# Expert and feed-forward layers of a fused attention and mixture-of-experts kernel: transposes by DMA and VectorE in place of the matmul engine, and the experts' second layer two blocks behind the first

## The reference

```
x = attention(q, k, v, a_re, a_im)              # decayed linear attention, 4 x 768 tokens, 8 heads of 48: x is 3072 x 384
e = argmax(x @ w_gate); gate = softmax(x @ w_gate)[e] * sigmoid(x @ w_output_gate)[e]     # 8 experts
y = gate * (relu(x @ w1[e]) @ w2[e])            # 384 -> 1024 -> 384, each token through one expert
h = y @ w_in;  out = max(0.01 * h, h) @ w_out   # 384 -> 2048 -> 384, all tokens
```

## Time and profile before

| | us |
|---|---|
| median of 3 runs (lowest, highest) | 1001.77 (1001.34, 1003.72) |
| the profiled execution's own time | 1002.58 |
| its span, first to last instruction | 1000.6 |
| PE busy | 949.9 (95%) |
| DVE, ACT, POOL busy | 412.9, 454.2, 509.5 |

### The profile page before, as it was taken

How to read it: one execution, slowest core, us unless ns; L and a number is a source line. 1 busy time by engine, 2 the same in 40 slices (tenths; PEclk the granted TensorE clock), 3 DMA queues, 4 the chain that set the end, 5 groups by cost and what they waited for, 6 DMA issues and landing times.

```text
span 1000.6 us, 17624 instructions
## 1 busy us (share of the span) xinstructions
PE 949.9 (95%) x5980; PEld 846.0 (85%) x5981; DVE 412.9 (41%) x742; ACT 454.2 (45%) x772; POOL 509.5 (51%) x429
## 2 busy tenths in 40 slices
PE   6999999999839999999999999999999999999997
PEld 5778788888727999998998989999999999999996
DVE  6889988988824323333232322212112122112111
ACT  7999889996612222222222333333333333333322
POOL 4235665665547558568839943243343332433433
PEclk9999999999968999999999999999999999999999
DMA  4643454320342343253535520010010010000000
GB/s 145 174 136 104 148 171 130 118 81 28 100 169 95 109 166 120 85 167 115 154 106 165 189 57 17 16 40 16 9 40 17 24 32 17 32 1 1 32 1 32
DMA packets 47192, 84.06 MB, mean 84 GB/s; under 512 B 23813, under 2 KB 36377, under 8 KB 44569
## 3 DMA queue, kind: packets, MB, share of 16 engines
q1 hardware_dynamic: 40984, 48.59, 16.3%
q0 software_dynamic: 6144, 34.65, 9.9%
HBM read 65.80 MB, written 17.38 MB: 83 GB/s over the span
## 4 chain that ended last, share of the span: by engine, by line
PE 74%; ACT 10%; DVE 5%; issue 5%; POOL 5%; SPq 1%; DMA 1%; POOLq 0%; DVEq 0%; ACTq 0%
PE bank L2127 20%; PE bank L2140 20%; PE bank L2085 11%; PE bank L2107 10%; POOL wm L1866 3%; PE bank L2095 2%; PE bank L1096 2%; DVE neglog L848 1%; PE bank L1178 1%; PE bank L1136 1%; POOL wm L1864 1%; PE bank L1164 1%; PE bank L1138 1%; PE bank L1106 1%; PE bank L1119 1%
## 5 line engine op out<-in xcount | busy, mean ns | idle before, releaser
L1894 POOL TENSOR_TENSOR act_r<-act_f,act_r 128x512 fp32r<-128x512 f32 x96 | 124.6, 1298 | 260.3 <-ACT act_r L1955 257.6
L2140 PE MATMUL bank<-w_out_r,act_r 128*128 128x384 f32 x1152 | 217.7, 337 | 0.3 <-POOL act_r L1894 0.3
L2127 PE MATMUL bank<-x,w_in_r 128*128 128x512 f32 x864 | 216.7, 395 | 0.0
L2140 PEld LDWEIGHTS bank<-w_out_r,act_r 128*128 128x128 f32 x1152 | 204.8, 188 | 8.8 <-POOL act_r L1894 0.6
L2016 DVE TENSOR_TENSOR act_f<-bank,small 128x512 f32<-128x512 f32 x96 | 66.5, 693 | 292.7 <-ACT small L1952 275.2
L2127 PEld LDWEIGHTS bank<-x,w_in_r 128*128 128x128 f32 x864 | 159.6, 188 | 29.5
L1952 ACT ACTIVATE small<-bank 128x512 f32<-128x512 f32 x96 | 57.5, 599 | 191.2 <-PE bank L2127 191.1
L2085 PE MATMUL bank<-wm,x_tr 128*128 (+1 forms) x522 | 129.5, 402 | 4.0 <-POOL wm L1866 1.7
L2107 PE MATMUL bank<-wm,h_tr 128*128 (+1 forms) x696 | 128.6, 339 | 0.7 <-DVE h_tr L2000 0.7
L2107 PEld LDWEIGHTS bank<-wm,h_tr 128*128 128x128 f32 x696 | 120.1, 188 | 0.9 <-issue 0.9
L2085 PEld LDWEIGHTS bank<-wm,x_tr 128*128 128x128 f32 x522 | 97.8, 192 | 25.1 <-issue 5.0
(11 more groups left out here) (195 smaller groups left out, 1406.4 us busy)
## 6 DMA issues: line engine op xcount, KB each, us to landing
stage<-moe_w POOLq DMA_DIRECT2D x12, 1536.0 KB, 7.0
qkv_in<-in_qkv SPq DMA_DIRECT2D x24, 576.0 KB, 6.0
a_in<-in_a SPq DMA_DIRECT2D x11, 768.0 KB, 5.1
stage<-moe_w SPq DMA_DIRECT2D x4, 1536.0 KB
x_b<-x_sorted SPq DMA_DIRECT2D x30, 193.0 KB
y_sorted<-y_b SPq DMA_DIRECT2D x29, 192.0 KB
xg<-y_sorted SPq DMA_DIRECT2D x24, 192.0 KB, 2.4
stage<-w_out POOLq DMA_DIRECT2D x2, 1536.0 KB, 7.3
```

The source lines that it names most:

```text
L1894: pool.tensor_tensor(a[:, 1, :], act_f[f % 2][:, :], a[:, 0, :].bitcast(F32), ALU.subtract).then_inc(s_gl, 1)
L2127: last = pe.matmul(h_bank[f % 2][:, :], w_in_r[:, wp, t * F2 + f * P:t * F2 + (f + 1) * P], window_part(w, xp)[:, t, :], start=(t == 0 and ...
L2140: last = pe.matmul(o_bank[j][:, 0:W], a[:, ap, j * P:(j + 1) * P], w_out_r[:, wp, f * W:(f + 1) * W], start=(f == 0 and n == 0), stop=(f = ...
```

## The change

- No transposes on PE. The rows come in by 4 DMAs per tile (`quarters`): quarter a of the 384 features of all 128 tokens goes to partitions 32a to 32a + 31, in runs of 96 values. VectorE then turns 32 x 32 squares into the same PSUM bank (`turn_tokens`, `turn` for the feed-forward tiles). The order of features that results is matched by the weights, which the host lays out by quarters (`by_quarter`).
- The hidden layer `h` goes to DRAM and back into `h_q` (`hidden_out`, `hidden_in`: 512 KB each way), and VectorE turns its squares in two instructions (`turn_hidden`).
- The gate is applied as the scale of the relu; it comes by a DMA of its own (`gates`).
- `layer2(g)` follows `layer1(g + 2)`. POOL's half 0 of an expert waits for `layer1` of the last block of expert e - 2, half 1 for its `layer2`.
- At the end PE runs `ff1(0, 0)` and `ff1(0, 1)` before the last block's `layer2`. ACT waits for that `layer2` before the first activation.

```diff
     def layers_sync(sp):
         def load(g):
-            sp.dma_start(x_b[:, :], xs[rows, :]).then_inc(s_xb, 16)
+            need(sp, s_tx, g)
+            rows = rows_of(g)
+            for a in range(Q):
+                sp.dma_start(x_q[a * SQ:(a + 1) * SQ, :].rearrange("i (b c) -> i b c", b=Q),
+                             quarters(xs[rows, 0:W], a)).then_inc(s_xb, 16)
+        def hidden_out(g):
+            sp.wait_ge(s_h, 2 * g + 2)
+            sp.dma_start(hs.rearrange("a t c -> t a c"), h[:, :].rearrange("t (a c) -> t a c", a=Q)).then_inc(s_hs, 16)
+        def hidden_in(g):
+            sp.wait_ge(s_hs, 16 * g + 16)
+            need(sp, s_hth, 2 * g)
+            sp.dma_start(h_q[:, :], hs.rearrange("a (i b) c -> (a i) (b c)", b=Q)).then_inc(s_hq, 16)
...
+        with sp.Fori(0, early) as g:
+            load(g + 4)
+            sp.wait_ge(s_hq, 16 * g + 32)
+            hidden_out(g + 2)
+            gates(g + 3)
+            hidden_in(g + 2)
             store(g)
...
     def layers_pool(pool):
-            if i == 0 and done is not None:
-                pool.wait_ge(s_p2, done)
+            if done is not None:
+                pool.wait_ge((s_p1, s_p2)[i], done)
...
     def layers_scalar(act):
         def relu(g):
+            act.wait_ge(s_gate_in, 16 * g + 16)
+            need(act, s_hs, 16 * g)
             act.wait_ge(s_p1, g + 1)
             for j in range(2):
-                act.activation(h[:, j * 512:(j + 1) * 512], hid_bank[j][:, :], ACT.Relu).then_inc(s_h, 1)
+                act.activation(h[:, j * 512:(j + 1) * 512], hid_bank[j][:, :], ACT.Relu,
+                               scale=gate_b[:, 0:1]).then_inc(s_h, 1)
...
+        leading(early + 3)
+        act.wait_ge(s_p2, early + 4)
         for f in range(2):
             hidden(f, f)
...
     def layers_vector(dve, route_vector, sorted_slots):
+        def turn_tokens(g):
+            dve.wait_ge(s_xb, 64 * g + 64)
+            need(dve, s_xl, g)
+            dve.transpose(tx_bank[:, 0:W].rearrange("p (k b i) -> p b k i", b=Q, i=SQ),
+                          x_q[:, :].rearrange("p (b k j) -> p b k j", b=Q, j=SQ)).then_inc(s_tx, 1)
+        def turn_hidden(g):
+            dve.wait_ge(s_hq, 16 * g + 16)
+            need(dve, s_hl, 2 * g)
+            for j in range(2):
+                dve.transpose(th_bank[j][:, :].rearrange("p (k i b) -> p b k i", b=Q, i=SQ),
+                              h_q[:, :].rearrange("p (b k j) -> p b k j", b=Q, j=SQ)[:, :, 4 * j:4 * j + 4, :]
+                              ).then_inc(s_hth, 1)
...
     def layers_tensor(pe):
-        with pe.Fori(1, last_g) as g:
-            transpose_hidden(g)
-            layer1(g + 1)
-            transpose_block(g + 2)
+        layer1(1)
+        layer1(2)
+        layer2(0)
+        with pe.Fori(1, before) as g:
+            layer1(g + 2)
             layer2(g)
-        layer2(last_g)
-        pe.wait_ge(s_wh, 2 * (E + 2))
-        ff1(0, 0)
-        ff1(0, 1)
+        layer2(before)
+        pe.wait_ge(s_wh, 2 * (E + 2))
+        ff1(0, 0)
+        ff1(0, 1)
+        layer2(last_g)
         windows(pe, body)
```

More of the change, by code:

```diff
@@ L1726, in late @@
         return t
-    x_b = nc.alloc_sbuf_tensor_at("x_b", [P, XR], F32, offset=masks_at)
+    x_q = nc.alloc_sbuf_tensor_at("x_q", [P, W], F32, offset=masks_at)
+    gate_b = sb(ctx, "gate_b", [P, 1])
     x_tr = sb(ctx, "x_tr", [P, 2, W], F32R)
     h = sb(ctx, "h", [P, F1])
+    h_q = sb(ctx, "h_q", [P, F1])
     h_tr = sb(ctx, "h_tr", [P, 2, F1], F32R)
@@ L1756, in experts_then_feed_forward @@
     s_ys = sem("block_stored")
-    s_in = [sem(f"tokens{i}_in") for i in range(TW)]
+    s_in = [sem(f"tokens{i}_in") for i in range(2)]
     s_tt = sem("tokens_transposed")
@@ L1843, in layers_sync @@
                      allow_slow_non_contiguous=True).then_inc(s_ids, 16)
-        for w in range(2, NW):
-            window(w)
+        for t in range(TW, NCH):
+            tile_in(t)
         for j in range(TW):
@@ L2020, in body @@
                 hidden(FT2 * w + f, f)
+                if f - 1 in AT and more:
+                    turn(w + 1, AT[f - 1])
                 if f - 2 in AT and more:
@@ L2032, in layers_vector @@
         dve.sem_inc(s_o, TW)
-        last_g = last_block(dve)
-        before = at(dve, T_LAST, 1, N // P - 2, NBMAX - 2)
+        early = third_before_last(dve)
+        turn_tokens(1)
         block_tokens(1)
+        turn_tokens(2)
+        block_tokens(2)
+        turn_hidden(0)
+        turn_tokens(3)
         trailing(0)
-        block_tokens(2)
+        block_tokens(3)
+        turn_hidden(1)
+        turn_tokens(4)
         result(0)
-        with dve.Fori(1, before) as g:
+        with dve.Fori(1, early) as g:
             trailing(g)
-            block_tokens(g + 2)
+            block_tokens(g + 3)
+            turn_hidden(g + 1)
+            turn_tokens(g + 4)
             result(g)
-        trailing(before)
-        block_tokens(before + 2)
-        result(before)
+        trailing(early)
+        block_tokens(early + 3)
+        turn_hidden(early + 1)
+        result(early)
         for j in range(2):
+            turn(0, j)
             tokens(0, j)
-        trailing(last_g)
+        trailing(early + 1)
+        turn_hidden(early + 2)
+        result(early + 1)
+        trailing(early + 2)
         for j in range(2, TW):
+            turn(0, j)
             tokens(0, j)
-        result(last_g)
+        turn_hidden(early + 3)
+        result(early + 2)
+        trailing(early + 3)
+        result(early + 3)
         for f in range(2):
@@ L2056, in layers_tensor @@
     def layers_tensor(pe):
-        def transpose_block(g):
-            pe.wait_ge(s_xg, g + 1)
-            need(pe, s_xl, g)
-            for j in range(KT):
-                last = pe.transpose(tx_bank[:, j * P:(j + 1) * P], x_b[:, j * P:(j + 1) * P], ident[:, :])
-            last.then_inc(s_tx, 1)
         def part_of(base, at_col, n):
@@ L2088, in layer1 @@
             last.then_inc(s_p1, 1)
-        def transpose_hidden(g):
-            for t in range(FT1):
-                if t % 4 == 0:
-                    pe.wait_ge(s_h, 2 * g + t // 4 + 1)
-                    need(pe, s_hl, 2 * g)
-                last = pe.transpose(th_bank[t // 4][:, (t % 4) * P:(t % 4 + 1) * P], h[:, t * P:(t + 1) * P],
-                                    ident[:, :])
-            last.then_inc(s_hth, 1)
         def layer2(g):
@@ L2155, in body @@
                     ff2(w, f)
-                if f in AT and more:
-                    transpose_token(w + 1, AT[f])
             if not more:
```

176 lines of the change are left out of this document (95 added, 81 removed).

## The result

| | before | after |
|---|---|---|
| median, us (lowest, highest) | 1002.19 (1001.34, 1003.72) | 1039.06 (1035.17, 1041.42) |
| ratio, 95% interval | | 1.0362 (1.0326 to 1.0399) |
| profiled execution, its span | 1002.58, 1000.6 | 1037.81, 1036.0 |
| PE busy | 949.9 | 928.5 |

The changed kernel is slower. I had forecast 968, with 960 to 988. The transposes did leave PE, but it is only 21 us less busy, since the matmuls of the experts' two layers took 273.4 us in place of 258.1, many of them at a lower clock behind a wait. The span grew by 35, so that PE now waits some 57 us more.

What follows compares the result with a forecast made beforehand. PE was taken as the bound in both parts. Span 1000.6 - 30.1 (up to `ff1(0, 2)`) - 6.6 (feed-forward transposes) + 2.9 (clock) = 966.8 us, 968.0 as median; range 960 to 988.

Steps and rivals of the forecast that it cites:

- Start: Start of the experts' part: `layer1(0)` starts at 300.33 us again, `layer1(2)` at 314.2.
- PE's part: Experts' blocks on PE: 8.38 us each without transposes, 1.14 us less than 9.52.
- VectorE: Transposes on VectorE cost as much as copies, 0.56 and 0.69 us; it has 5.0 us of work in 8.38.
- Rival C: VectorE is the bound, its transposes costing over 5.4 us a block; 1027 us at four times a copy; chance 0.03.
- Duration of the transfers: Hidden layer through DRAM, 512 KB each way: 3.3 us out and 3.0 us in.
- the loop of 6.9 us: SP's loop of hidden-layer write and read, with 0.6 us of hand-overs; 8.2 us averaged with weight loads, inside 8.38.
- The crossings: `stage` weight loads delay the hidden layer's transfers by up to about 4 us, 14 times in 21 blocks; averaged 1 to 1.5 us a block.
- the slack of two blocks: From the end of `layer1(g)` to `layer2(g)` 16.8 us, leaving about 4 us of slack for late transfers.
- The end: Before the feed-forward part: PE waits 5.3 us for weights, the clock costs 2.9 us; `ff1(0, 2)` at 560.0 without the latter.
- The feed-forward part: 20 tiles lose 0.33 us of PE transposes each, 6.6 us in all.
- Rival B: Hidden layer's DRAM loop sets the pace, slower result above 9.9 us a block; at 11.2 us, 1039 us; chance 0.06.

Runs made afterwards that it cites:

- run 1: The changed kernel without the 16 later weight loads into stage, the splits kept: 985.72 us, ratio 0.9809.
- run 3: The changed kernel with a block's tokens loaded by one DMA of whole rows in place of four by quarters: 1015.39 us, ratio 1.0107.
- run 8: run 5 with VectorE copying a block's result before it transposes the next tokens: 1005.31 us, ratio 1.004.
- run 2: The changed kernel with the hidden layer transposed on PE again, no way through DRAM, second layer one block behind: 991.77 us, ratio 0.9882.
- run 9: run 8 with the hidden layer written and read in two halves of 256 KB: 1021.66 us, ratio 1.0185.
- run 10: run 8 with each block's gates loaded along with its tokens, into a column of their own: 1016.36 us, ratio 1.0112.
- run 4: The changed kernel with SP's issues reordered and a place in DRAM for each block's hidden layer: 1037.37 us, ratio 1.0334.
- run 5: The changed kernel with ScalarE issuing the hidden layer's transfers on its own queue, a place in DRAM for each block: 1037.19 us, ratio 1.0334.
- run 7: run 2 with the first four feed-forward tiles loaded earlier and two of them turned earlier: 988.82 us, ratio 0.9855.

## Why the prediction was wrong

In the order of its steps, against the span of 1036.0 (forecast 966.8, 69.2 us less):

- *Start.* `layer1(2)` at 314.2, measured 316.11: 1.9 us.
- *PE's part.* 8.38 us for a block without transposes is right; the blocks of run 1 outside its three dips show it.
- *VectorE.* 0.56 and 0.69 us a transpose, measured 0.59 and 0.70. Rival C had no ground. The Trainium skill's 311 ns for 128 x 128 in bf16 ("VectorE: DVE Perf Modes", "The three transpose paths"), from which I worked out 3.4 us a block, doesn't carry over: 2.0 us were measured in float32.
- *Duration of the transfers.* Write 3.3 taken, 2.94 measured where nothing crosses; read 3.0 taken, 3.4 to 3.5 measured.
- *The step that failed:* the loop of 6.9 us that "averaged" comes to "8.2 us: inside 8.38, but hardly", for which "I count nothing". It was wrong in four places. SP's own 5 us a block, which I put "while a transfer is under way", lie beside the read, but in series with the write: 2.94 + 4.98 = 7.92 us, not 6.9 (run 3 takes three issues out and 1.6 us with them). The crossings cost 2.8 us a block, not 1 to 1.5; the prediction's own figures, 14 times about 4 us over 21 blocks, give 2.7, and nothing there says why only half of it was taken. Part of the 2.8 are the small scatters, which the prediction doesn't have at all: without weight loads 0.47 us a block is left on PE (run 1). And the slack of two blocks was set against a mean: slack takes up a single late transfer, it can't take up a loop that is longer than the pace for good. A loop of 7.92 has only 0.46 us a block below 8.38 to work the crossings off. That gives 10.71 us a block from write to write and 10.78 on PE, from block 2 to 28 62.3 us too much.
- *The end.* From `layer1(28)` to `ff1(0, 2)` I had 30.8 us, with 5.3 for weights and 2.9 for the clock; measured 36.4 (596.31 to 632.71). The weights came in time because the blocks were late. In their place stand the waits for `h_tr` of blocks 26 and 27, 9.79 and 1.35 us, and the clock did fall, behind the first of them: `layer2(26)` took 6.68 us in place of 4.2. 5.6 us.
- *The feed-forward part.* 403.3 us from `ff1(0, 2)` to the end, 403.9 forecast. The 6.6 us of transposes are gone.

The sum: 1.9 + 62.3 + 5.6 - 0.6 = 69.2.

Rival B named the right loop and the bound of 9.9 us. That its price fits (11.2 us a block against 10.78, and 1039) is luck: it was made of 5.3 us for each way and 0.6, and measured were 2.94 for a write that nothing crosses, 5.2 to 8.3 for a crossed one, 4.98 of SP's work, and the read for the most part beside it. I gave it 0.06, because a block's own small loads were quick. They were no evidence: the trace before has little beside them. The row that was evidence, 576 KB in 6.0 us with other loads beside it, I called an upper end. What was also missing in the working is the plain sum of DMA time: 25.8% and 14.5% of 220 us from the trace before, and for the new 1 MB some 3.3 us a block, as run 8 shows (95 us for 29 blocks). By itself it wouldn't have given the result, as the 7.7 us of the changed kernel are below 8.38.

What is shown: without the weight loads the loss is gone (run 1), without the hidden layer's way too (run 2); with the same bytes, issued by ScalarE and with another order on VectorE, 34 us of the 37 are gone (run 8), so the bytes alone don't make it. That order is the reason, and not ScalarE's queue or the places in DRAM, is argued from the loops and not shown. What stays open: why the same bytes in halves cost 16 us (run 9), and which part of 1005 against run 1's 986 is order and which the DMA engines at 79%. Runs 9 and 10 were to open a further loop and lost, but each brings a cost of its own, so they don't settle it.

## What to carry to other kernels

When work moves from an engine to DMA, first add up the DMA engines' time per step, old and new, and then walk each loop: every transfer, wait and issue from one write to the next on the same queue and buffer, with the largest transfer that can cross it charged in full. Slack covers a late step, never a mean above the pace; and a wait taken out of one in-order queue can turn up in the next (runs 4, 5 and 10), so open all queues of the loop together. Take the part whose transfers have room (the tokens here, 1.4% faster in run 7) and leave the other on the matmul engine.

## What the runs showed of the hardware

- A transfer's time under crossing has little to do with its size: 0.5 KB took 9.88 us (run 10), 512 KB 5.2 to 8.8 us, where they take 1.8 (median of run 2) and 2.9 to 3.5 us by themselves (chain of the changed kernel, medians of run 1).
- Small scatters also count: in run 1, with no weight loads at all, a token load took 6.57 us while POOL's scatters of 4-byte entries ran, against 1.9 us in the median, and four writes of 512 KB took 5.8 to 7.6 us, against 3.0.
- VectorE's square transposes of float32 into PSUM cost about a copy: 592 ns for 384 columns, where the copy of `y_b` takes 540, and 704 for 512.
- A relu with a scale from a column takes 685 ns, the kernel before's without it 596. The Trainium skill, "ScalarE: Activation LUTs", section "What ACT_TABLE_LOAD costs", gives some 93 ns for such an operand; this agrees.
- The clock: after PE's waits of 3.7 and 9.8 us at the end of the experts the next `layer2` took 6.81 and 6.68 us in place of 4.2, and in 610 to 616 us the granted clock was 0.55, the lower of its two levels for most of the stretch:

```profile
610.00:616.00 6.00, 5.54 (x19) 5.54 (x20) 2.22 (x4) 1.82 (x4) 0.00 (x0) 0.55 0.51 141
```
